# Delta-rule attention with two feed-forward layers: lane weights of the first chunk from the keys, its solve in blocks of eight, triangles scaled on VectorE, loads reordered

## The reference, cut to what matters

```python
k_n = k / (norm(k) + 1e-6)               # q, k, v: (4, 8, 768, 48); beta: (4, 8, 768)
for t in range(768):                     # per (batch, head), state S: (48, 48)
    y[t] = q[t] @ S
    S = S + beta[t] * outer(k_n[t], v[t] - k_n[t] @ S)
x = y.transpose(0, 2, 1, 3).reshape(3072, 384)
h = relu(x @ w_in); x = (h * h) @ w_out                            # w_in 384 x 2048
out = (silu(x @ w_gate) * (x @ w_val)) @ w_out2                    # 384 x 1536 each
```

## Time and profile before

| | |
|---|---|
| median of 3 runs | 1029.84 us |
| the runs | 1026.11, 1029.84, 1029.98 us |
| the profiled execution | 1026.33 us |
| its span | 1024.6 us |
| PE, DVE, ACT, POOL busy | 990.8, 409.6, 308.5, 229.2 us |
| PE from 440 to 1020 us | busy 579.83 of 580 us |
| PE's mean granted clock | 0.985 of full speed |

### The profile page before, as it was taken

How to read it: one execution, slowest core, us unless ns; L and a number is a source line. 1 busy time by engine, 2 the same in 40 slices (tenths; PEclk the granted TensorE clock), 3 DMA queues, 4 the chain that set the end, 5 groups by cost and what they waited for, 6 DMA issues and landing times.

```text
span 1024.6 us, 25035 instructions
## 1 busy us (share of the span) xinstructions
PE 990.8 (97%) x11096; PEld 822.7 (80%) x11096; DVE 409.6 (40%) x677; ACT 308.5 (30%) x602; POOL 229.2 (22%) x385
## 2 busy tenths in 40 slices
PE   6589989999999999999999999999999999999998
PEld 5578889778778787877888888888888888888886
DVE  4676544543643644443366322322322322323222
ACT  2255334332433423332355311211211212212211
POOL 2795680780582185000000000000000000000000
PEclk9699899999999999999999999999999999999999
DMA  7757566356245333511173100100100100100000
GB/s 216 216 176 206 151 179 159 85 151 160 86 110 153 91 103 110 127 57 37 32 239 100 63 1 1 61 1 1 62 1 1 62 1 0 63 1 1 31 1 31
DMA packets 120699, 85.20 MB, mean 83 GB/s; under 512 B 94416, under 2 KB 99920, under 8 KB 120592
## 3 DMA queue, kind: packets, MB, share of 16 engines
q1 hardware_dynamic: 110448, 75.68, 26.3%
q10 hardware_dynamic: 10144, 7.93, 2.6%
HBM read 62.88 MB, written 20.71 MB: 82 GB/s over the span
## 4 chain that ended last, share of the span: by engine, by line
PE 92%; DVE 2%; DMA 2%; issue 1%; ACT 1%; ACTq 1%; SPq 1%; DVEq 0%
PE bank L1231 91%; DMA small_tri_scratch<-gram 1%; DVE h_lo L1190 1%; DMA w_spare<-in_w 1%; DMA k_dim<-in_kt 0%; ACT h_hi L930 0%; ACT gram L955 0%; ACT w_hi L930 0%; PE bank L1464 0%; DVE w_lo L1169 0%; DVE u_tok L1146 0%; ACTq L579 0%; DMA small_inv_scratch<-small_inv 0%; ACTq L591 0%; SPq L601 0%
## 5 line engine op out<-in xcount | busy, mean ns | idle before, releaser
L1231 PE MATMUL bank<-x_hi,w_hi 128*128 128x512 f32 (+1 forms) x768 | 293.8, 383 | 0.0
L1231 PE MATMUL bank<-x_lo,w_hi 128*128 128x512 f32 (+1 forms) x768 | 289.6, 377 | 0.0
L1231 PE MATMUL bank<-x_hi,w_lo 128*128 128x512 f32 (+1 forms) x768 | 289.4, 377 | 0.0
L1231 PE MATMUL bank<-h_hi,w_hi 128*128 128x512 f32 (+1 forms) x552 | 211.4, 383 | 6.3 <-DVE h_lo L1190 5.6
L1231 PE MATMUL bank<-h_hi,w_lo 128*128 128x512 f32 (+1 forms) x552 | 205.7, 373 | 0.0
L1231 PE MATMUL bank<-h_lo,w_hi 128*128 128x512 f32 (+1 forms) x552 | 205.6, 373 | 0.0
L1210 DVE TENSOR_TENSOR stage<-bank,stage 128x512 f32<-128x512 f32 x72 | 49.8, 692 | 318.4 <-ACT stage L1049 318.4
L1231 PEld LDWEIGHTS bank<-x_hi,w_hi 128*128 128x128 f32 x768 | 145.3, 189 | 27.7
L1231 PEld LDWEIGHTS bank<-x_hi,w_lo 128*128 128x128 f32 x768 | 145.3, 189 | 26.4
L1231 PEld LDWEIGHTS bank<-x_lo,w_hi 128*128 128x128 f32 x768 | 145.4, 189 | 25.3
L1184 DVE TENSOR_TENSOR stage<-stage,bank 128x512 f32<-128x512 f32 (+1 forms) x112 | 68.4, 611 | 193.2 <-ACT stage L1021 193.1
(11 more groups left out here) (124 smaller groups left out, 600.9 us busy)
## 6 DMA issues: line engine op xcount, KB each, us to landing
w_raw<-in_w SPq DMA_DIRECT2D x12, 576.0 KB, 3.8
k_dim<-in_kt SPq DMA_DIRECT2D x12, 512.0 KB, 4.3
q_dim<-in_qt SPq DMA_DIRECT2D x12, 512.0 KB, 3.6
x1s<-in_w ACTq DMA_DIRECT2D x14, 384.0 KB, 4.3
k_sq<-in_ky SPq DMA_DIRECT2D x12, 384.0 KB, 3.7
v_tok<-in_vy SPq DMA_DIRECT2D x12, 384.0 KB, 3.5
x_in<-x_scratch SPq DMA_DIRECT2D x6, 768.0 KB, 5.0
out<-out_sb SPq DMA_DIRECT2D x18, 256.0 KB, 2.4
```

What stands on the lines that cost most here:

```text
L1231: return pe.matmul(dst, lhsT, rhs, start=start, stop=stop, **kw)
```

## The change

The first chunk's lane weights no longer come from the diagonals of the stored blocks. A new input kl holds the keys with one lane per partition; DVE squares and sums it (stage norms), and ACT takes the root (small lane 0). The load of ky(0) moves behind `load_small(0)`. `small_solve` for n = 0 works on the two 8 x 8 diagonal blocks together in 7 steps and joins them with two products over 512 elements and two sums. DZ 0 accumulates onto U 0 in its banks, with the residual taken out negated, and is shared by ACT and DVE as a plain copy. The scaling of the triangles moves from POOL's `solve` to a DVE stage (triangles), behind each lane stage. The hand-written orders change, two w1 stages move by one slot, and four calls in SP's order move.

```diff
@@ orders of the first pass
-                       ("U", 0): (1, 2), ("Z", 0): (3, 4), ("DZ", 0): (7, 0), ("Y", 0): (1, 2), ("DS", 0): (3, 4),
-                       ("X", 0, 0): (7,), ("X", 0, 1): (0,)}
-        ACT_FIRST = [("G", 0), ("quarters", 0), ("sq", 0), ("G", 1), ("G", 2), ("quarters", 1), ("G", 3), ("root", 0),
-                     ("small lane", 0), ("fetch", 1), ("fetch", 2), ("tri", 3), ("w1", 0), ("w1", 1), ("w1", 2),
-                     ("small lane", 1), ("inv", 0), ("fetch", 3), ("fetch", 4), ("E", 0), ("L", 0), ("lane", 1),
-                     ("w1", 3), ("U", 0), ("w1", 4), ("Z", 0), ("sq", 1), ("back", 1), ("fetch", 5), ("fetch", 6),
-                     ("Y", 0), ("X", 0, 0), ("X", 0, 1), ("E", 1)]
-        DVE_FIRST = [("G", 0), ("G", 1), ("S", 0), ("G", 2), ("root", 0), ("G", 3), ("small lane", 0), ("solve", 0),
-                     ("small lane", 1), ("S", 1), ("scale", 0), ("w1", 0), ("w1", 1), ("E", 0), ("L", 0), ("QK", 0),
-                     ("U", 0), ("lane", 1), ("Z", 0), ("w1", 2), ("DZ", 0), ("w1", 3), ("w1", 4), ("Y", 0), ("DS", 0),
-                     ("X", 0, 0), ("X", 0, 1), ("E", 1)]
+                       ("U", 0): (1, 2), ("Z", 0): (3, 4), ("DZ", 0): (1, 2), ("Y", 0): (7, 0), ("DS", 0): (3, 4),
+                       ("X", 0, 0): (1,), ("X", 0, 1): (2,)}
+        ACT_FIRST = [("G", 0), ("quarters", 0), ("small lane", 0), ("G", 1), ("G", 2), ("quarters", 1), ("G", 3),
+                     ("fetch", 1), ("fetch", 2), ("sq", 0), ("tri", 3), ("w1", 0), ("w1", 1), ("w1", 2),
+                     ("small lane", 1), ("root", 0), ("inv", 0), ("fetch", 3), ("fetch", 4), ("E", 0), ("L", 0),
+                     ("lane", 1), ("U", 0), ("w1", 3), ("Z", 0), ("w1", 4), ("sq", 1), ("DZ", 0), ("back", 1), ("Y", 0),
+                     ("fetch", 5), ("fetch", 6), ("X", 0, 0), ("X", 0, 1), ("E", 1)]
+        DVE_FIRST = [("G", 0), ("norms", 0), ("G", 1), ("small lane", 0), ("S", 0), ("G", 2), ("G", 3), ("solve", 0),
+                     ("small lane", 1), ("root", 0), ("S", 1), ("scale", 0), ("w1", 0), ("w1", 1), ("E", 0), ("L", 0),
+                     ("QK", 0), ("U", 0), ("lane", 1), ("Z", 0), ("triangles", 1), ("w1", 2), ("DZ", 0), ("w1", 3),
+                     ("w1", 4), ("Y", 0), ("DS", 0), ("X", 0, 0), ("X", 0, 1), ("E", 1)]
@@ plan(0), and a triangles stage behind each lane stage
-                for f, slot in zip(range(RING + SPARE, NF1), (2, 4, 6, 8, 10, 12, 14, 16, 19, 22, 25)):
+                for f, slot in zip(range(RING + SPARE, NF1), (3, 4, 6, 8, 10, 12, 15, 16, 19, 22, 25)):
                 put(29, "lane", 2)
+                put(29, "triangles", 2)
                         put(3 if t == 2 else 1, "lane", p)
+                        put(3 if t == 2 else 1, "triangles", p)
@@ solve (POOL)
-            eng.wait_ge(tri_loaded, 16 * t)
-            eng.wait_ge(lane_step, 5 * (t + 2))
-            then(eng.tensor_tensor(a[:, :, :], a[:, :, :], lane_nw[:, :].unsqueeze(1).to_broadcast([P, HALF, HALF]),
-                                   ALU.mult))
+            eng.wait_ge(tri_scaled, t)
@@ small_solve, n == 0
+                ad, xd = eighths(small_tri[0]), eighths(small_inv[0])
+                scaled = lane_nw[:, weights].rearrange("p (b i) -> p b i", b=2)
+                then(eng.tensor_tensor(ad, ad, scaled.unsqueeze(2).to_broadcast([P, 2, EIGHTH, EIGHTH]), ALU.mult))
+                then(eng.tensor_scalar(a[:, 0:EIGHTH, EIGHTH:SMALL], a[:, 0:EIGHTH, EIGHTH:SMALL], -1.0, None, ALU.mult))
+                then(eng.tensor_copy(diagonal(x, SMALL), lane_w[:, weights]))
+                for j in range(EIGHTH - 1):
+                    block = [P, 2, EIGHTH - 1 - j, j + 1]
...
+                    then(eng.tensor_tensor(share, ad[:, :, j, j + 1:EIGHTH].unsqueeze(3).to_broadcast(block),
+                                           xd[:, :, j:j + 1, 0:j + 1].to_broadcast(block), ALU.mult))
...
+                    then(eng.tensor_tensor(below, below, share, ALU.add))
...
+                then(eng.tensor_tensor(share, a[:, 0:EIGHTH, EIGHTH:SMALL].rearrange("p k i -> p i k").unsqueeze(2)
+                                       .to_broadcast(cube),
+                                       x[:, 0:EIGHTH, 0:EIGHTH].rearrange("p k c -> p c k").unsqueeze(1).to_broadcast(cube),
+                                       ALU.mult))
+                then(eng.tensor_reduce(mid, share, AX.X, ALU.add))
+                then(eng.tensor_tensor(share, x[:, EIGHTH:SMALL, EIGHTH:SMALL].unsqueeze(2).to_broadcast(cube),
+                                       mid.rearrange("p k c -> p c k").unsqueeze(1).to_broadcast(cube), ALU.mult))
+                then(eng.tensor_reduce(x[:, EIGHTH:SMALL, 0:EIGHTH], share, AX.X, ALU.add))
@@ SP's order
             load_k(0)
+            sp.dma_start(k_sq[:, :, :].rearrange("p h d -> p (h d)"), kl[0]).then_inc(keys_loaded, 16)
             sp.dma_start(rest[0][:, :, :, :].rearrange("p r m t -> p (r m t)"), kt[2]).then_inc(ahead_loaded[0], 16)
-            load_ky(0)
             sp.dma_start(beta_sb[:, :, :], beta).then_inc(beta_loaded, 16)
             store_quarters(sp, 0, (0, 1))
             load_small(0)
+            load_ky(0)
             load_v(0)
             load_q(0)
...
             load_k(4)
-            load_ky(5)
             load_x(2)
+            load_q(4)
+            store_y(3)
             load_prep(7)
             store_both(6)
-            load_q(4)
-            store_y(3)
             store_inverses(2)
+            load_ky(5)
             load_ktok(4)
@@ ACT: the roots of small lane; DVE: norms and triangles
+                    squares = lane_t[:, at] if n == 0 else diagonal(small_tri[n][:, 0:SMALL, :], SMALL)
+                    act.activation(lane_t[:, at], squares, ACT.Sqrt).then_inc(lane_root, 1)
...
+                elif name == "norms":
+                    dve.wait_ge(keys_loaded, 16)
+                    dve.tensor_tensor(k_sq[:, :, :], k_sq[:, :, :], k_sq[:, :, :], ALU.mult).then_inc(keys_squared, 1)
+                    dve.wait_ge(keys_squared, 1)
+                    dve.tensor_reduce(lane_t[:, 0:SMALL], k_sq[:, :, :], AX.X, ALU.add).then_inc(keys_summed, 1)
+                elif name == "triangles":
+                    dve.wait_ge(tri_loaded, 16 * n)
+                    dve.tensor_tensor(tri[:, :, :], tri[:, :, :], lane_nw[:, :].unsqueeze(1).to_broadcast([P, HALF, HALF]),
+                                      ALU.mult).then_inc(tri_scaled, 1)
@@ Z and DZ of chunk 0: out negated, then accumulated onto U
+                (minus if n == 0 else copy)(resid[:, part, :, :, :].rearrange("p r a d -> p (r a d)"), bank[:, 0:8 * D]
+                                            ).then_inc(z_ready[part], 1)
+            elif name == "DZ":
+                copy(u_tok[:, part, :, :].rearrange("p m d -> p (m d)"), bank[:, 0:8 * D]).then_inc(u_ready, 1)
...
-                                              resid[late(ab), bp, r, a, :])
+                                              resid[late(ab), bp, r, a, :], start=(n > 0), skip_group_check=(n == 0))
```

More of the change, by code:

```diff
@@ L3, with program @@
 from contextlib import ExitStack
-def program(nc, kt, qt, kz, ky, vy, beta, w1, w2, out):
+def program(nc, kt, qt, kz, ky, kl, vy, beta, w1, w2, out):
     f32 = mybir.dt.float32
@@ L192, in program @@
         lane_root = sem("lane_root")
+        keys_loaded = sem("keys_loaded")
+        keys_squared = sem("keys_squared")
+        keys_summed = sem("keys_summed")
+        tri_scaled = sem("tri_scaled")
         lane_step = sem("lane_step")
@@ L464, in w1_place, with take_out @@
             return x1s[:, k % RING, :], w1_loaded[k % RING], 2 + k // RING
-        def take_out(copy, stage_, part):
+        def take_out(copy, stage_, part, minus=None):
             name, n = stage_
@@ L532, in small_solve @@
         def small_solve(eng, n):
-            a, x, products, steps = small_tri[n], small_inv[n], small_prod[n], small_step[n]
+            a, x = small_tri[n][:, 0:SMALL, :], small_inv[n][:, 0:SMALL, :]
+            products, steps = small_prod[n], small_step[n]
             at = [0]
@@ L545, in small_solve @@
             eng.wait_ge(lane_step, 5 * (n + 1))
-            then(eng.tensor_tensor(a[:, :, :], a[:, :, :], lane_nw[:, weights].unsqueeze(1).to_broadcast([P, SMALL, SMALL]),
-                                   ALU.mult))
-            then(eng.tensor_copy(diagonal(x, SMALL), lane_w[:, weights]))
-            for j in range(SMALL - 1):
+            if n == 0:
+                ad, xd = eighths(small_tri[0]), eighths(small_inv[0])
[5 more added lines that the diff above has]
+                    block = [P, 2, EIGHTH - 1 - j, j + 1]
+                    share = eighth_prod[:, 0:2 * block[2] * block[3]].rearrange("p (b i c) -> p b i c", b=2, c=block[3])
+                    then(eng.tensor_tensor(share, ad[:, :, j, j + 1:EIGHTH].unsqueeze(3).to_broadcast(block),
```

(23 more changed lines are left out.)

42 lines of the change are left out of this document (26 added, 16 removed).

## The result

| | before | changed |
|---|---|---|
| median of 7 runs each | 1029.84 us (1026.11 to 1033.15) | 1022.95 us (1022.46 to 1025.90) |
| measured again (35 and 12 runs) | 1027.97 us (1024.10 to 1032.95) | 1023.47 us (1019.92 to 1026.12) |
| ratio, first and second comparison | 1 | 0.9948 (0.9930 to 0.9967), 0.9954 (0.9934 to 0.9974) |
| profiled execution (span) | 1026.33 (1024.6) | 1025.36 (1023.6); second 1020.16 (1018.4) |

A forecast was written before the change was run, and what follows sets the result against it. PE, busy 97% of the span, was taken as the bound, so only its gaps and half-clock time count. Terms -0.7 -2.0 -2.6 -4.2 +0.2 = -9.3 took 1026.33 to 1017.0, plus 3.5 to the median: 1020.5 us, range 1014 to 1027.5.

The forecast's parts named there:

- The moved loads: Unit 1, Y 3: later loads and triangle stores remove PE's stop and clock drop, -4.2; G 7's wait for k_prep, +0.2.
- rival 1: Y 3: the gap is not from the burst, so the 4.2 stays; 1024.7 us, chance 0.20.
- the rule named from the Trainium skill: Y 3: instruction fetch is hidden by the pace of issue, so moved loads free nothing; sum 4.2 smaller.
- rival 3: G 7 becomes the wait: k_prep lands as late as 9.6 us, PE waits 4.8; 1025 us, chance 0.12.
- The clock at 114 us: After unit 0's h_lo gap: half of the 2.9 us lost to the half-speed clock comes back, -1.4.
- What the triangles brought: Triangles scaled on DVE: h_lo wait -0.7, clock after it -1.4, waits at 270 and 357 us -0.5; together -2.6.
- Unit 0's slots: Unit 0: two w1 loads moved past h_lo shorten PE's waits, -1.0 each, together -2.0 (0 to -2.4).
- The first chunk: To 53 us: later loads +0.8, E 0 path +0.2, earlier Z 0 -1.2, DZ copy -0.5; sum -0.7.
- The solve at nothing: First chunk: inverse ready about 2.6 us earlier, counted as nothing because SP's queue covers it; solve 6.8 against 7.9.
- The distance of 3.5 us between profile and median: Median of runs 1029.84 against profiled 1026.33; the difference was added to 1017.0, giving 1020.5.
- Rival 2: First chunk: quarter stores land sooner, the inverse comes through and the clock returns earlier, another -3.5; 1017.0 us, chance 0.17.
- rival 4: Slower: unit 0 meets the half-speed clock for twice 13 us, +13.2; 1033.7 us, chance 0.06.

The follow-up runs named there:

- the seven: Seven traces with the changed kernel's first pass: two of the changed kernel, five of variants leaving that pass's loads and stores alone; no single time.
- the three of before: Three traces of kernels with the first pass of before, set against traces with the changed first pass; no single time.
- the first chunk's part alone: Only the first chunk's part of the change; slots, POOL's scaling and SP's unit 1 order as before: 1028.03 against 1028.21 us, ratio 0.9988.

## Why the prediction was right or wrong

By sign and range it held; the amount was some 4 us too large. The stated time, 1020.5, came nearer (2.5 to 3) than the amount, by luck: the median of three runs from which it starts, 1029.84, was 1.6 to 2.0 above those of the three later sets (24 to 35 runs). The parts by ratio: first chunk -1.2, triangles -1.5, slots -1.7, loads 0 to -0.9, together -4.4 to -5.3, against -5.0 for the whole. They add up, but each alone is uncertain by 2 to 3 us, so this can't show whether one part spoils another.

- **The moved loads (-4.2 +0.2), the step that failed.** Its cause was read rightly: the stop comes and goes with the burst, and the block's transfer is late with it (rival 1 and the rule named from the Trainium skill fell), the clock at 148 came back, and k_prep landed in 5.9 us. G 7's wait was 0.8 to 1.1, not 0.2: rival 3 in small. In unit 1 the term measures -3.3. What was missing is what the new order does further on. The prediction treated one stop; the boundaries recur, and one of the next, at x3624, met the queue's later orders and stopped PE for 1.0 us in the mean, most of the 1.6 that came back. The sentence that the other shorter "issue" gaps stay was the wrong one. Net -1.6 by traces and 0 to -0.9 by ratios, instead of -4.0.
- **The clock at 114 us (-1.4).** It did not come. PE's wait did shrink as foreseen (1.24 to 0.34, and the two of 0.35 went), but a stop at a block boundary lies in the same place, and the clock fell to its lower level all the same: for 3.4 us there in most traces, with either engine; the 6.8 of the first trace were long for either. What the triangles brought, 1.5, is the sum without this term, 1.2, within the error. It lies elsewhere than foreseen: in the table of unit 1, the stretch behind it is 1.5 (old order) and 1.3 (new order) shorter with DVE's scaling, and the two waits are 0.7 of that.
- **Unit 0's slots (-2.0).** -1.7 by ratio; of the two gains the second was mostly turned into G 5's wait, and PE's waits fell by 1.2. In the traces unit 0 is 1.3 shorter in the mean (new slots and DVE's scaling: 64.87, 61.99, 62.01, 63.74, 63.22, 61.65; the three with the first pass of before: 63.79, 66.09, 62.64).
- **The first chunk (-0.7).** -1.2 by ratio; by traces the first feed-forward work starts 0.85 earlier (54.27 against 55.12). Its terms, in means of the seven against three: the load of the small triangles 0.96 later (+0.8 forecast), E 0 1.1 later (+0.8 and +0.5), from U 0 to Z 0 0.8 shorter (-1.2), DVE's u_tok ahead of Y 0.86 instead of 1.32 (-0.5). Then a stop at x728, in the middle of DZ, was 1.4 long against 0.45, and one at x979 (0.5 to 2.0) went. One term is missing in the prediction: L 1 at the head of unit 0 needs chunk 1's inverse, whose last load was issued 1.9 to 3.7 us ahead of the unit in the three of before and in the first chunk's part alone, and from 1.3 us ahead of it to 0.1 behind in the other six of the seven. L 1 waits 0.7 in the mean of the seven (0 to 1.8) and never in the three. Most of the 0.85 went there.
- **The solve at nothing** was right, and for the reason given: 15 steps cost the same. It took 7.4 us, not 6.8.
- **The distance of 3.5 us between profile and median** was carried along as if it belonged to the kernel. It is the draw: later medians of the kernel before are 1027.9 to 1028.2.
- Rival 2 did not come (the store went out at 27.0 to 28.4); nor did rival 4 (no new long stretch at half clock).

What stays open: what the stop at x1241 is; why one execution has longer stops than another; whether a change so small that it only shifts the boundaries would do as much as the moved loads, which was not tried.

## What to carry to other kernels

A PE stop without a releaser, in straight-line code and at the same matmul count in every execution, may be a late block of instructions; the instruction queue's transfers tell, as one then lands just before PE goes on. Move the loads that fill the DMA engines before it, and then look at the next boundaries under load, because what the queue issues later moves too. Where a stall is removed, ask for each engine's queue what it had been covering (here root 0 and S 1 behind the stores, the keys' squares behind h_lo, chunk 1's inverse behind the first chunk). Where such stops vary by several microseconds, take several traces of each kernel before subtracting two.

## What the runs showed of the hardware

An instruction block of 16 KB was in PE's hands 1.2 to 1.7 us after its transfer landed, in all 91 stops. A product of 512 elements over two operands in SBUF, read with axes exchanged or repeated, took 1.01 and 1.10 us on DVE, where the line through the two smaller ones gives 0.73. And where 384 KB stand ahead of small stores in SP's order, the load behind these goes out 0.96 us later (means of seven and three traces; 1.7 by the one trace in which only these 384 KB and ACT's squares were moved); 896 KB (v and q) taken from ahead of them brought it 3.2 us earlier (25.25 to 22.06).
